# Attention and expert kernel on one core: similarities of the next pair moved behind the second score, first centroid columns and mask rows made first, one rounding moved to GpSimd

## The reference

```python
q, k, v: (2, 8, 768, 64)     centroids: (8, 16, 64)
q_assign = argmax(einsum('bhsd,hcd->bhsc', q_n, c_n))   # nearest centroid of each query
k_assign = argmax(einsum('bhsd,hcd->bhsc', k_n, c_n))   # and of each key
mask = q_assign[..., :, None] == k_assign[..., None, :]
scores = where(mask, scale * q @ k.T, -1e9)
out = softmax(scores) @ v
# then x = out as 1536 rows of 512; one of 8 experts for each row (w_gate, w1, w2),
# and last (x @ w_a) * (x @ w_b) @ w_out
```

## Time and profile before

| | us |
|---|---|
| median of three runs | 818.38 |
| the three runs | 825.77, 818.35, 818.38 |
| the profiled execution | 825.37 |
| its span, from the first instruction to the last | 823.60 |
| TensorE busy in the span | 813.3 |
| VectorE, ScalarE, GpSimd busy | 455.9, 362.3, 363.9 |

### The profile page before, as it was taken

The page is one execution under the profiler, slowest core; times in us unless marked ns, Lnnn a source line. Parts: engine busy times, 40 slices in busy tenths (PEclk is TensorE's granted clock), DMA queues, the critical chain, the costliest instruction groups (busy, mean ns, idle before and its releaser), DMA issues.

```text
span 823.6 us, 13160 instructions
## 1 busy us (share of the span) xinstructions
PE 813.3 (99%) x4409; PEld 685.9 (83%) x4410; DVE 455.9 (55%) x711; ACT 362.3 (44%) x742; POOL 363.9 (44%) x305
## 2 busy tenths in 40 slices
PE   7999999999999999999999999999999999999997
PEld 4999999999998688888888888888888888888886
DVE  5689879879888898999767103631211112121211
ACT  7578778778787433434434443111112112121112
POOL 6558988988985264544535644000321002010001
PEclk9699999999999999999999999999999999999999
DMA  7434534534423376887767412400101000010001
GB/s 192 115 95 138 146 95 137 143 99 138 101 80 118 109 246 213 240 256 247 223 200 231 147 40 78 140 1 14 26 13 53 1 14 13 1 52 0 1 1 51
DMA packets 48632, 86.58 MB, mean 105 GB/s; under 512 B 17840, under 2 KB 19888, under 8 KB 48592
## 3 DMA queue, kind: packets, MB, share of 16 engines
q1 hardware_dynamic: 41888, 69.36, 29.3%
q0 software_dynamic: 3824, 11.29, 4.6%
q10 hardware_dynamic: 2880, 5.39, 1.7%
HBM read 73.25 MB, written 11.30 MB: 103 GB/s over the span
## 4 chain that ended last, share of the span: by engine, by line
PE 79%; issue 15%; DMA 2%; POOL 1%; DVE 1%; ACT 1%; POOLq 0%; SPq 0%; DVEq 0%
PE bank L1585 9%; PE bank L1653 9%; PE bank L1419 8%; PE bank L1552 7%; PE bank L1554 6%; PE bank L1553 6%; PE bank L1390 4%; PE bank L1590 4%; PE bank L1409 4%; PE bank L1657 4%; PE bank L1435 4%; PE bank L1437 3%; PE bank L1447 2%; PE bank L1351 2%; PE bank L1597 2%
## 5 line engine op out<-in xcount | busy, mean ns | idle before, releaser
L1315 DVE TENSOR_TENSOR ab_raw<-bank,a_sb 128x512 f32<-128x512 f32 x35 | 24.2, 692 | 187.6 <-PE bank L1554 187.6
L1101 DVE TENSOR_REDUCE neg_max<-bank 128x1 f32<-128x768 f32 x96 | 91.4, 953 | 36.1 <-PE bank L1409 35.9
L398 DVE CAST w_split<-stage 128x1024 fp32r<-128x1024 f32 x68 | 66.5, 978 | 73.2 <-PE bank L1590 53.8
L402 DVE TENSOR_TENSOR w_split<-stage,w_split 128x1024 fp32r<-128x1024 f32 x72 | 102.4, 1425 | 2.3
L825 ACT ACTIVATE pT_hi<-bank 128x384 fp32r<-128x384 f32 x192 | 84.9, 491 | 40.6 <-PE bank L1419 38.2
L1069 DVE TENSOR_TENSOR pT_lo<-bank,pT_hi 128x384 fp32r<-128x384 f32 x192 | 98.0, 550 | 4.1 <-ACT pT_hi L825 3.6
L693 POOL TENSOR_TENSOR hT_lo<-hT_raw,hT_hi 128x512 fp32r<-128x512 f32 x38 | 55.7, 1467 | 82.0 <-ACT hT_raw L897 81.7
L845 ACT ACTIVATE probs<-bank,neg_max 128x768 f32<-128x768 f32 x96 | 87.0, 907 | 10.8 <-DVE neg_max L1101 10.7
L1419 PE MATMUL bank<-ident,probs 128*128 128x128 f32 x576 | 83.1, 281 | 0.4 <-DVE pT_lo L1069 0.4
L957 ACT ACTIVATE a_sb<-bank 128x512 f32<-128x512 f32 x35 | 20.9, 597 | 134.8 <-PE bank L1554 134.8
L1653 PE MATMUL bank<-w_split,hT_hi 128*128 (+1 forms) x304 | 79.4, 403 | 0.0
(11 more groups left out here) (250 smaller groups left out, 1743.5 us busy)
## 6 DMA issues: line engine op xcount, KB each, us to landing
stage<-w SPq DMA_DIRECT2D x64, 512.0 KB, 4.6
q_raw<-qT SPq DMA_DIRECT2D x32, 192.0 KB, 3.7
k_raw<-kT SPq DMA_DIRECT2D x32, 192.0 KB, 3.9
sorted_y<-y_sb ACTq DMA_DIRECT2D x19, 257.0 KB, 4.8
q_pair<-qT SPq DMA_DIRECT2D x8, 384.0 KB, 4.4
v_raw<-v_keys SPq DMA_DIRECT2D x16, 192.0 KB, 3.7
stage<-w_a SPq DMA_DIRECT2D x6, 512.0 KB, 4.6
stage<-w_b SPq DMA_DIRECT2D x6, 512.0 KB, 4.5
```

Of the source, the lines that this page charges most:

```text
L402: eng.tensor_tensor(dst[:, 1], stage[:, i % STAGES], dst[:, 0].bitcast(F32), ALU.subtract).then_inc(s_cv, 1)
L1101: dve.tensor_reduce(neg_max[:, qt % 2:qt % 2 + 1], scores[qt % 2][:, 0:S], AX_X, ALU.max, negate=True).then_inc(s_max, 1)
```

## The change

- The transposed centroids go to PSUM bank 4 in place of bank 7. VectorE first copies the columns of pair 0 alone (two copies of 64 rows by 16 columns), then the other three pairs of the first batch and the four of the second, in four copies. The similarities of pair 1 wait for all six (`s_cTs`).
- VectorE's query mask rows (L1182) are copied in two pieces, 256 and 512 columns; the third score waits for the second piece.
- The high part of the second head's queries is made by GpSimd in place of ScalarE.
- ScalarE lays the gate weights (L809) after the exponential of the second head's first tile, not before the mask rows.
- The similarities of pair 1 stand behind the second score (six tiles), in turn 2 (three) and in turn 3 (three).
- Filler matmuls: two in place of four behind the transposed centroids, five in place of four ahead of the first high-order scores, none (three before) between those and the one-hot transposes, three in place of four behind these.

```diff
--- before.py
+++ after.py
@@ -641,6 +641,8 @@
             pool.wait_ge(s_qk[1], 64)
             pool.wait_ge(s_khm, 1)
             pool.tensor_tensor(k_hm[0:D, 1], k_raw[0:D, 1], one[0:D], ALU.mult).then_inc(s_khm, 1)
+            pool.wait_ge(s_qhh, 1)
+            pool.tensor_tensor(q_hh[:, 1], q_raw[:, 1], scale, ALU.mult).then_inc(s_qhh, 1)
             pool.wait_ge(s_qhh, 2)
             pool.wait_ge(s_qs, 1)
             pool.tensor_tensor(q_raw[0:D, 1], q_raw[0:D, 1], scale[0:D], ALU.mult).then_inc(s_qs, 1)
@@ -794,19 +796,21 @@
                 rows = slice(half * D, half * D + D)
                 act.activation(back_w[rows, :, 0:D], ident[rows, rows].unsqueeze(1).to_broadcast([D, G, D]), ACT.Copy).then_inc(s_bw, 1)
 
-            def first_highs(g):
+            def first_key_high(g):
                 act.wait_ge(s_qk[g], 64)
                 act.activation(k_hl[:, g], k_raw[:, g], ACT.Copy).then_inc(s_khi, 1)
-                act.activation(q_hh[:, g], q_raw[:, g], ACT.Copy, scale=float(D) ** -0.5).then_inc(s_qhh, 1)
-
-            first_highs(0)
+
+            first_key_high(0)
+            act.activation(q_hh[:, 0], q_raw[:, 0], ACT.Copy, scale=float(D) ** -0.5).then_inc(s_qhh, 1)
             act.wait_ge(s_qhh, 1)
             act.activation(q_raw[0:D, 0], q_raw[0:D, 0], ACT.Copy, scale=float(D) ** -0.5).then_inc(s_qs, 1)
             act.activation(k_hm[0:D, 0], k_raw[0:D, 0], ACT.Copy).then_inc(s_khm, 1)
-            first_highs(1)
-            act.wait_ge(s_back_w, 32)
-            for b in range(B):
-                act.activation(back_w[:, b * H:(b + 1) * H, D:XW], gate_w[:, :, :], ACT.Copy).then_inc(s_bw, 1)
+            first_key_high(1)
+
+            def lay_gate_weights():
+                act.wait_ge(s_back_w, 32)
+                for b in range(B):
+                    act.activation(back_w[:, b * H:(b + 1) * H, D:XW], gate_w[:, :, :], ACT.Copy).then_inc(s_bw, 1)
 
             def make_mask_rows(pp):
                 act.wait_ge(s_hotT, pp + 1)
@@ -847,6 +851,8 @@
                                    accum_out=row_sum[:, slot, qt, 0:1]).then_inc(s_exp, 1)
                     if qt % GT == 1 and (not static(g) or g >= 1):
                         copy_oT(g - 1, qt // GT)
+                    if first and (slot, qt) == (1, 0):
+                        lay_gate_weights()
                     if more and slot == 1 and qt == (3 if first else 2):
                         make_mask_rows(pp + 1)
 
@@ -1032,11 +1038,14 @@
             dve.tensor_scalar(cen_rows[:, :, :], cen_rows[:, :, :], cen_n[:, 7:8], None, ALU.mult).then_inc(s_cunit, 1)
             dve.wait_ge(s_set, 8)
             dve.wait_ge(s_cT, 1)
+            unit_T = bank[:, 4, 0:P].rearrange("d (j two c) -> d j two c", two=2, c=C)
             for two in range(2):
                 rows = slice(two * D, two * D + D)
-                unit_T = bank[rows, 7, 0:P].rearrange("d (j two c) -> d j two c", two=2, c=C)[:, :, two, :]
-                dve.tensor_copy(cen_pair[rows, :, two, :].rearrange("d (b j) c -> d b j c", b=B),
-                                unit_T.unsqueeze(1).to_broadcast([D, B, H // 2, C])).then_inc(s_cTs, 1)
+                dve.tensor_copy(cen_pair[rows, 0, two, :], unit_T[rows, 0, two, :]).then_inc(s_cTs, 1)
+            for two in range(2):
+                rows = slice(two * D, two * D + D)
+                dve.tensor_copy(cen_pair[rows, 1:H // 2, two, :], unit_T[rows, 1:, two, :]).then_inc(s_cTs, 1)
+                dve.tensor_copy(cen_pair[rows, H // 2:, two, :], unit_T[rows, :, two, :]).then_inc(s_cTs, 1)
 
 
             def assign(pp, step):
@@ -1179,7 +1188,8 @@
                 dve.tensor_tensor(one_hot[:, 2 + half * n:2 + half * n + n, 0:C], c_minus_ps[:, 0:n, :], by_c(first_idx),
                                   ALU.is_equal).then_inc(s_asgn, 1)
             dve.wait_ge(s_hotQ, 1)
-            dve.tensor_copy(q_lm[D:D + C, 0], first_hot_T[D:D + C, :]).then_inc(s_qm0, 1)
+            for cols in (slice(0, 2 * P), slice(2 * P, S)):
+                dve.tensor_copy(q_lm[D:D + C, 0, cols], first_hot_T[D:D + C, cols]).then_inc(s_qm0, 1)
             over_pairs(dve, pair)
             evacuate(G * QT - 2, QT - 2)
             row_norm(G - 1, (G - 1) % 2)
@@ -1341,8 +1351,8 @@
             pe.wait_ge(s_const, 2)
             spin(9)
             pe.wait_ge(s_cunit, 1)
-            pe.transpose(bank[:, 7, 0:P], cen_rows[:, :, :].rearrange("p two d -> p (two d)"), ident[:, :]).then_inc(s_cT, 1)
-            spin(4)
+            pe.transpose(bank[:, 4, 0:P], cen_rows[:, :, :].rearrange("p two d -> p (two d)"), ident[:, :]).then_inc(s_cT, 1)
+            spin(2)
 
 
             def sim_rows(pp, t, out):
@@ -1352,6 +1362,8 @@
 
             def similarities(pp, tiles):
                 if tiles[0] == 0:
+                    if static(pp) and pp == 1:
+                        pe.wait_ge(s_cTs, 6)
                     pe.wait_ge(s_pair, 32 * (pp + 1))
                     pe.wait_ge(s_hotr, pp)
                 for t in tiles:
@@ -1395,6 +1407,8 @@
                     score_high(g, slot, qt)
                 at = slice(qt * P, (qt + 1) * P)
                 ps = scores[qt % 2]
+                if static(n) and n == 2:
+                    pe.wait_ge(s_qm0, 2)
                 if qt == 0:
                     pe.wait_ge(s_qlm, g + 1)
                     pe.wait_ge(s_khm, g + 1)
@@ -1453,7 +1467,7 @@
                 more = not static(pp) or pp + 1 < PAIRS
                 before = not static(g) or g >= 1
                 first = static(pp) and pp == 0
-                sim_tiles = {qt: range(4 * qt - 8, 4 * qt - 4) for qt in (2, 3, 4)} if first else {0: range(6), 1: range(6, 12)}
+                sim_tiles = {1: range(6), 2: range(6, 9), 3: range(9, 12)} if first else {0: range(6), 1: range(6, 12)}
                 for qt in range(QT):
                     n = g * QT + qt
                     score(pp, g, n, slot, qt)
@@ -1509,12 +1523,11 @@
             pe.wait_ge(s_cTs, 2)
             first_similarities(0)
             first_similarities(1)
-            spin(4)
+            spin(5)
             score_high(0, 0, 0)
             score_high(0, 0, 1)
+            first_hot_transposes()
             spin(3)
-            first_hot_transposes()
-            spin(4)
             over_pairs(pe, pair)
             N = G * QT
             transpose_probs(N - 2, 0)
```

## The result

| | before | after |
|---|---|---|
| median, 20 executions each | 825.69 us | 820.32 us |
| lowest, highest | 818.15, 829.62 | 816.00, 820.99 |
| profiled execution (span) | 825.37 (823.6) | 820.99 (819.2) |

The ratio is 0.9937, with a 95% interval from 0.991 to 0.9963: faster by 0.6%, inside the 1% that a measurement of this kernel tells from no change, but outside the range that I gave. The median of before is no longer 818.38: of all 92 timed executions of the kernel before in this study (without two disturbed ones), 14 lie between 818.1 and 819.0 us and 78 between 823.6 and 829.6. Of the 20 of the changed kernel, 8 lie between 816.0 and 816.6 us and 12 between 819.2 and 821.0. The first three runs of before held two of its rare low kind.

The account below looks back on a forecast made before the run. TensorE, busy 99% of the span, and its clock were taken as the bound. 825.37 - 1.0 (mask rows) - 0.7 (emptier turns) - 6.99 (no half-clock hole) = 816.7 us; range 815.4 to 818.9.

Parts of the forecast that it names:

- the median as an execution without a loss: Reading 818.38 us as an execution without the half-clock stretch, the profiled 825.37 as one with it, 6.99 us apart.
- the hole: Stretch of TensorE at 1.2 GHz in the profiled execution, from about 19.57 to 36.63 us: 17.1 us.
- Fewer falls: TensorE's idle gap before the third score shrinks from 1.71 to 0.5 us, so the clock should fall less often.
- rival 1: The clock falls in the median execution too: 822.1 us, up to 824.4; decides if over half have the hole; chance 0.13.
- My sign of being right: Among the signs of a right forecast: granted clock 1.00 throughout, with no half-clock stretch between 18 and 37 us.
- The sum without losses: Median 818.38 less 1.0 (mask rows) and 0.7 (emptier turns): 816.7 us, 0.2% less.
- Part 1: Centroid columns: two 64x16 copies first, taken at 0.13 us each, move the similarities 0.33 us earlier (bounds 0 and 0.6).
- Parts 2 and 3: One-hot transposes 0.5 us earlier; ScalarE's new order starts mask rows at 13.9, low-order scores at 15.05: 1.0 us earlier.
- Part 4: Moved work: GpSimd's query highs (1.47 us) delay split values to 24.4 us; gate weights 0.39 us; all hidden, nothing charged.
- Part 5: Next pair's similarities moved: turns 2 to 4 go from 6.75 to 5.88 us, 0.9; 0.7 taken, something off for start-up.
- Rival 2: The moved similarities are worth nothing since VectorE and ScalarE pace the first head anyway: 817.4 us; chance 0.15.
- The page on the clock: Skill page holding that only gaps longer than any here cost the clock; the prediction disagreed, citing 1.71 us before the fall.

Follow-up runs that it names:

- early: Changed kernel with 13 opening filler matmuls in place of nine, begun at about 1.3 us, not 2.05: ten executions 815.96 to 816.53 us, two at 820.43 and 821.93.
- both: Changed kernel with the opening filler begun at about 1.3 us plus filler matmuls in turn 1: nine executions 816.25 to 816.58 us, ratio to before 0.9918.
- filler: Changed kernel with filler matmuls in turn 1, two ahead of the six similarity tiles and one behind every two: 816.5 to 817.5 us in five, 820.7 to 821.3 in three.

## Why the prediction was wrong

**The step that failed: the median as an execution without a loss.** From three runs I read 818.38 as the rule and 825.4 as the exception, and let the clock's part drop out of the comparison; the slow start stands in the sum at nothing, because I hadn't seen it. The runs showed that of 92 executions of the kernel before 78 have a loss, and of 27 of the changed kernel 16: 8 slow starts and 8 falls. The two middle executions of the 20 that give the median, 820.31 and 820.32 us, have a mean clock of 1.000: by my sorting they are slow starts, 4.1 us above 816.2, the middle one of the low values. Rows 2 and 6 already spoke against the reading of before: the only profiled execution had the hole, behind an idle stretch of 1.71 us that nothing in the kernel makes rare.

**Fewer falls, as said.** Mean clocks show 64 falls in 72 executions before and 8 in 27 after. So rival 1, the fall in the median execution, was not the case by its own condition, more than half of the executions with the hole: in the result it is 5 of 20. It looked right, since the time came out on its side, but slow starts put it there. My sign of being right, a granted clock of 1.00 throughout, fits the median executions too, and could not have told.

**What rival 1 had mis-sized.** I priced it at 822.1 to 824.4 us, and the falls came out at 820.7. I took 1.0 and 2.3 us out of a hole of unchanged length. The hole became 7 us shorter; the new places of the similarities alone did as much, in the one trace of them (10.3 us).

**A loss that I did not see.** The slow start was in the profile of before in part:

```profile
2.05 4.01 PE L1339 MATMUL bank<-ident_bf 128*128 128x512 bf16 x9 [2.05 <-POOL ident_bf L564]
```

Nine fillers take 4.01 us there, 0.43 us from start to start, while others take 0.22. I read the strip of the granted clock, which says full speed, and not the durations. Of the changed kernel's 27 executions 8 are slow starts, near 820.6 us, and worth 4.3 us each.

**The sum without losses was near.** 816.7 was forecast, and the low values are 816.0 to 816.6 against 818.1 to 819.0: 2.2 us between their middle ones, 1.7 forecast.
- *Part 1*: from the centroids' transpose to the first similarity 1.20 us before and 0.96 after, so 0.24 in place of 0.33. The two 64x16 copies take 0.19 us each, not 0.13. The similarities began at 7.64 and not 7.4 us, partly since the transpose itself was 0.13 us later in that execution.
- *Parts 2 and 3*: transposes 13.45 (13.35 forecast), key mask rows 14.05 (13.9), low-order scores 15.18 (15.05), third score 17.84 (17.7). The gain is 0.9 of the 1.0 us, and undoing ScalarE's part costs 1.15. VectorE's two casts were through by 15.4 us and nothing waited for them.
- *Part 4*: GpSimd's rounding takes 1.46 us, the values are split at 24.6 (24.4 forecast), and TensorE waits for neither. Hidden, as said.
- *Part 5*: the tiles ran from 16.2 to 17.7. The turns at full clock are read from VectorE's row maxima, here with the early filler and the change:

```profile
18.75 0.96 DVE L1110 TENSOR_REDUCE neg_max<-bank 128x1 f32<-128x768 f32 x1 [1.22 <-PE bank L1425]
...
20.78 0.96 DVE L1110 TENSOR_REDUCE neg_max<-bank 128x1 f32<-128x768 f32 x1
...
22.81 0.96 DVE L1110 TENSOR_REDUCE neg_max<-bank 128x1 f32<-128x768 f32 x1
...
24.61 0.95 DVE L1110 TENSOR_REDUCE neg_max<-bank 128x1 f32<-128x768 f32 x1
```

and here in the kernel before with filler alone:

```profile
19.78 0.96 DVE L1101 TENSOR_REDUCE neg_max<-bank 128x1 f32<-128x768 f32 x1 [1.22 <-PE bank L1411]
...
22.03 0.96 DVE L1101 TENSOR_REDUCE neg_max<-bank 128x1 f32<-128x768 f32 x1 [0.37 <-PE bank L1411]
...
24.28 0.96 DVE L1101 TENSOR_REDUCE neg_max<-bank 128x1 f32<-128x768 f32 x1 [0.37 <-PE bank L1411]
...
26.54 0.96 DVE L1101 TENSOR_REDUCE neg_max<-bank 128x1 f32<-128x768 f32 x1 [0.37 <-PE bank L1411]
```

The three turns last 2.03, 2.03 and 1.80 us against 2.25, 2.25 and 2.26: 5.86 against 6.76, which is the 0.9 us of the working. The 0.2 us that I took off for the start-up were not lost. The idle 0.37 us of VectorE in each old turn show that TensorE set the pace, and their absence shows that VectorE nearly does now. Rival 2 is refuted by that, and by the changed kernel with the old places, whose low value is 1.0 us higher. The new places alone moved the low value of the kernel before by 0.6 us only; why not by 0.9 stays open.

**The page on the clock.** The Trainium skill (TensorE: Matmul & The Clock Gate, Why this matters for your kernels) would have left the clock up over such gaps. The runs disagree. Behind 1.71 us of idleness it fell in most executions: of the 72 of the kernel before whose mean clock was recorded, 64 are slow, each with 0.988 to 0.992. With filler in the gap (and a longer opening filler) it fell in none of five. Nor does a short gap keep it up: in the changed kernel's trace it fell with no gap over 0.24 us in the 10 us before. Whether it falls depends on the execution, and no run here shows what differs from one execution to the next.

**Left open.** The slow start is as common in the changed kernel (8 of 27) as the fall (8 of 27). Slow starts of any length seem about as frequent before (23 of 92, by their times), but the short ones near 826.8 us have no counterpart after. Whether the change made slow starts longer, by its two fillers fewer behind the centroids' transpose, was not tried apart; with two opening fillers, four of ten executions of the kernel before got the clock up at about 10 us, judging by their times and the one trace, and none of ten of the changed kernel; that points this way.

## What to carry to other kernels

When the runs of one kernel fall into values several microseconds apart, find out which kind the profiled execution is and forecast how often each kind occurs, not only what a good execution costs; three runs don't tell. Read matmul durations as well as the granted clock. Ahead of work that sets the end, an idle TensorE was not free here: filler matmuls that need no data, in the stretch of 1 to 2 us in which it idled and from as early as some constant tile existed, left no loss in 14 executions of two kernels. Real work in the same stretch did not do that: with the similarities there, seven of eleven and 8 of 27 executions had a fall. Where a fall can come, try to keep such work out of the turns behind it too: in the traces here the half-clock stretch ended only behind the last of it.

## What the runs showed of the hardware

- TensorE starts at 1.2 GHz in every execution traced here: nine fillers of 512 columns take 3.5 to 4.0 us from 2.04 us on, at first 0.43 us from one to the next, where 0.22 is usual later. Up to the first fall the granted clock nevertheless reads 1.00, and an execution with 15 us at half speed has a mean clock of 1.000. Matmul durations are the witness for the start of a trace.
- Nine opening fillers left 8 of 27 executions of the changed kernel at half clock until 17 us; thirteen, begun 0.6 us earlier, left none of 21 (the kernels "early" and "both"), by time and mean clock.
- Once down, the clock stayed down through turns in which TensorE was busy all the time: for 17.1 or 13.7 us with four similarity tiles in each of three turns, 10.2 with three in two turns, 3.4 with none.
- The clock fell behind an idle stretch of 1.71 us (64 of 72 executions), and also where similarities filled that stretch (7 of 11, and 8 of 27 in the changed kernel). With filler matmuls there it fell in none of 22 (the kernels "filler", "both" and the kernel before with filler).
